# A gated-MLP mixture's u product by one level of Strassen, in 7 of 8 batches

## The chip, the cores and the metric

The kernel runs on one core of one Trainium2 chip. The metric is the device time of one execution in microseconds, the median of the runs shown. "Profile" and "trace" are the record of one such execution.

## What is computed

Attention without a softmax over 8 batches, 8 heads, 576 rows of 64, with an RMS norm; a first mixture (a low-rank token mix, and a channel MLP 512 to 2048 to 512 with ReLU); then the second mixture, which this text is about:

```python
def _moe2_ref(x, w_in, g_ln, w_sg, b_sg, w_out):      # x: 8 x 576 x 512
    h = x @ w_in                                      # 512 x 1024
    h = gelu_tanh(h)
    u, v = (h[..., :512], h[..., 512:])
    v_n = (v - mean(v)) / np.sqrt(var(v) + 1e-06) * g_ln
    v_s = np.einsum('ts,bsd->btd', w_sg, v_n) + b_sg[None, :, None]
    gated = u * v_s
    return (x + gated @ w_out)
```

## The kernel before

Every product in float32 precision is made of three matmuls (`product`, L1611): each operand is split into a high and a low part (ScalarE copies the high one with rounding, VectorE or GpSimd subtracts it for the low one), and hi x hi, hi x lo and lo x hi are summed in PSUM. In the listing of the trace these are L1613, L1614 and L1615.

The first mixture's two big products (to about 836 us) already use one level of Strassen. The second mixture runs batch after batch (b = 2p + par, par the parity). TensorE's order in `iteration` (L1921) is: v product of batch b (`v_product`, tiles of 128 rows, 12 matmuls of 512 columns each; 5 tiles where par is 0, 4 where it is 1, since the 64 rows left over of two batches share a tile), output product of batch b - 1 (`out_product`, 4 tiles while b is odd, 5 while it is even, two banks by turns, so tile i + 2 waits until VectorE has evacuated tile i), u product of batch b (`u_product`: 4 column blocks of 128, 2 halves of 288 rows, 4 chunks), spatial product (`spatial`: 4 column blocks, 28 matmuls of 288 columns each).

The other engines run fixed queues beside it, and a queue is strict: an instruction that waits holds up what is behind it.

- ScalarE: `v_part` (gelu of each v tile into v_act, a ring of three; then the high part vn_hi of the tile before), then in `iteration` (L1075) `x2_high` of the next batch's x, the gelu of u's four column blocks out of PSUM into u_act, and the high parts ga_hi of the gated product.
- VectorE: `v_part` (L1500: statistics of tile j, `normalise` of tile j - 1, `low` of tile j - 2; at its end, behind the last normalise, the evacuation of the output product's tile 0), `evacuate_others`, `x2_transposed` (L1558: transposes xt_in blocks into o_st for the residual), `gate` (L1536: per column block the scale and bias out of PSUM into vs, the mult by u_act, and the low part ga_lo of the block before).
- GpSimd: `inverse_std` per v tile, `x2_low` of the next batch (L765).
- SyncE issues the transfers; `next_batch` (L697) has, in this order: first three xt_in blocks of this batch, the load of the next batch's x (`load_x2`), the output stores of the batch before (each waits for its evacuation), the two tail transfers, the other xt_in blocks (each waits until a buffer has been transposed).

x2_hi and x2_lo stand in two buffers, one per parity; x2_raw, the float32 x, in one. In batch 0 the same steps stand outside the loops, together with the transposes of w_sg.

Of the kernel before, what the change touches and what calls it, by code (L numbers as in the profile page):

```python
# [4 lines left out]
F32 = mybir.dt.float32  # L5
# [5 lines left out]
P = 128  # L11
# [108 lines left out]
def build(nc, q, k, v, g_norm, U, V, w_ch1, w_ch2, w_in, g_ln, w_sg, b_sg, w_out, out):  # L120
# [102 lines left out]
    x2_hi, x2_lo = [None, None], [None, None]  # L223
    o_st = [None] * NO
    cursor[0] = low + 24576
    x2_raw = at("x2_raw", [P, DC, NJ * P], F32)
# [6 lines left out]
    vs = at("vs", [P, 2, S], F32)  # L233
    assert cursor[0] <= hi_off[2]
    cursor[0] = low + 57344
    u_act = at("u_act", [P, DC, S], F32)
    o_st[0] = at("o_st0", [P, D], F32)
    assert cursor[0] <= hb_off[2]
    cursor[0] = hb_off[2]
    x2_lo[0] = at("x2_lo0", [P, DC, NJ * P], F32R)  # L240
    o_st[1] = at("o_st1", [P, D], F32)
    x2_hi[0] = at("x2_hi0", [P, DC, NJ * P], F32R)
# [11 lines left out]
    bias_bc = at("bias_bc", [P, S], F32)  # L254
    assert cursor[0] <= hb_off[1]
# [3 lines left out]
    x2_hi[1] = at("x2_hi1", [P, DC, S], F32R)  # L259
    x2_lo[1] = at("x2_lo1", [P, DC, S], F32R)  # L260
# [3 lines left out]
    with ExitStack() as ctx:  # L264
# [44 lines left out]
        s_x2l, s_x2hi, s_x2lo, s_x2lof = [sem(f"x2_loaded{i}") for i in range(2)], sem("x2_hi_ready"), sem("x2_lo_ready"), sem("x2_lo_first")  # L309
# [62 lines left out]
        def ws_tile(j, n=S):  # L372

            o = (2, 0)[j % 2] * 512
            return psf[:, o:o + n]

# [21 lines left out]
        def _(sp):  # L398
# [174 lines left out]
            def load_x2(p, par):  # L573

                t = (2 * p + par) * S
                if not isinstance(p, int) or p > 0:
                    sp.wait_ge(s_x2lo, 2 * p + par - 1)
                elif par:
                    sp.wait_ge(s_x2lof, 1)
                sp.dma_start(x2_raw[:, :, 0:S], x2T_dram[:, :, bass.ds(t, S)]).then_inc(s_x2l[par], 16)  # L580
                if par == 0:
                    sp.dma_start(x2_raw[:, :, S:], x2T_dram[:, :, bass.ds(t + S + SM, ST)]).then_inc(s_x2l[0], 16)
# [91 lines left out]
            load_x2(0, 0)  # L674
# [16 lines left out]
            load_x2(0, 1)  # L691
# [27 lines left out]
        def _(pool):  # L719
# [45 lines left out]
            def x2_low(p, par):  # L765
                n = (NJ * P, S)[par]
                pool.wait_ge(s_x2hi, 2 * p + par + 1)
                nc.gpsimd.tensor_tensor(x2_lo[par][:, :, 0:n], x2_raw[:, :, 0:n], x2_hi[par][:, :, 0:n].bitcast(F32),
                                        ALU.subtract).then_inc(s_x2lo, 1)
# [21 lines left out]
        def _(act):  # L791
# [91 lines left out]
            def x2_high(p, par, first=False):  # L883
                n = (NJ * P, S)[par]
                act.wait_ge(s_x2l[par], (32, 16)[par] * (p + 1))
                if not first:
                    act.wait_ge(s_umm, DC * (2 * p + par - 1))
                nc.scalar.activation(x2_hi[par][:, :, 0:n], x2_raw[:, :, 0:n], ACT.Copy).then_inc(s_x2hi, 1)


# [156 lines left out]
            def down_tile(t, first=False, last=False):  # L1047
                for n in range(NQ if first else 0, NSL):
                    if first and n in W2_AT:
                        w2_high(W2_AT[n])  # L1050
                    if n == 2 * NQ:
                        first_copied(t)
                    if n < 2:
                        h_relu(t, n + 2)
                    elif n >= NSL - 2 and not last:
                        h_relu(t + 1, n - NSL + 2)
                    if last and n == NSL - 2:
                        x2_high(0, 0, first=True)
# [13 lines left out]
            def us_tile(n):  # L1072
                return ps[:, 4 + 2 * (n % 2):6 + 2 * (n % 2), 0:SH]

            def iteration(p, par, first=False, last=False):  # L1075
                b = 2 * p + par
                if not first and not last:
                    x2_high(*after(p, par))
                for c in range(DC):
                    act.wait_ge(s_umm, DC * b + c + 1)  # L1080
                    if not first:
                        act.wait_ge(s_ga, DC * (b - 1) + c + 1)
                    nc.scalar.activation(u_act[:, c, :].rearrange("p (a m) -> p a m", a=2), us_tile(c),
                                         ACT.Gelu_apprx_tanh).then_inc(s_uact, 1)
                    for j in (WS_AFTER[c] if first else ()):
                        act.wait_ge(s_wsT, j + 1)
                        nc.scalar.activation(ws_hi[:, j, :], ws_tile(j), ACT.Copy).then_inc(s_wshi, 1)
                if first:
                    x2_high(*after(p, par), first=True)
# [44 lines left out]
        def _(dve):  # L1134
# [330 lines left out]
            def x2_low(p, par):  # L1465
                dve.wait_ge(s_x2hi, 2 * p + par + 1)
                for c in range(DC):
                    ins = nc.vector.tensor_tensor(x2_lo[par][:, c, :], x2_raw[:, c, :], x2_hi[par][:, c, :].bitcast(F32), ALU.subtract)
                ins.then_inc(s_x2lof, 1)
# [26 lines left out]
            x2_low(0, 0)  # L1496
# [36 lines left out]
            def us_tile(n):  # L1533
                return ps[:, 4 + 2 * (n % 2):6 + 2 * (n % 2), 0:SH]
# [37 lines left out]
            def evacuate_others(p, par, start=1):  # L1572
                for i in range(start, batch_tiles(par)):
                    evacuate(p, par, i)

# [12 lines left out]
            gate(0, 0, first=True)  # L1588
            with dve.Fori(0, B // 2 - 1) as i:
                v_part(i, 1)  # L1590
                evacuate_others(i, 0)
                x2_transposed(i, 1)
                gate(2 * i + 1, 1)
                v_part(i + 1, 0)
                evacuate_others(i, 1)
                x2_transposed(i + 1, 0)
                dve.wait_ge(s_ost[JM], 32 * (i + 1))
                gate(2 * i + 2, 0)
            v_part(B // 2 - 1, 1)
            evacuate_others(B // 2 - 1, 0)  # L1600
            x2_transposed(B // 2 - 1, 1)
            gate(B - 1, 1)
            for i in range(batch_tiles(1)):
                evacuate(B // 2 - 1, 1, i, bank=i)
# [3 lines left out]
        def _(pe):  # L1608
# [209 lines left out]
            def v_product(p, par, first=False):  # L1818
                if first:
                    pe.wait_ge(s_x2lof, 1)  # L1820
                else:
                    pe.wait_ge(s_x2lo, 2 * p + par)
                for j in range(VB[par], VB[par + 1]):
# [3 lines left out]
                    for c in range(DC):  # L1827
                        ins = product(ps[:, j % 2], [x2_hi[par][:, c, js], x2_lo[par][:, c, js]],
# [16 lines left out]
            def last_out_product(p, par):  # L1845
                tiles = batch_tiles(par)
                for c in range(DC):
                    pe.wait_ge(s_galo, DC * (2 * p + par) + c + 1)
                    for i in range(tiles):
# [5 lines left out]
                        ins = product(ps[:, i], [ga_hi[:, c, js], ga_lo[:, c, js]], [wo_hi[:, c, :], wo_lo[:, c, :]],  # L1855
# [16 lines left out]
            def u_product(b, par, first=False):  # L1872
                for c in range(DC):
                    if c < 2:
                        if not first:
                            pe.wait_ge(s_vs, DC * b + c - 1)
                    else:
                        pe.wait_ge(s_uact, DC * b + c - 1)
                    for h in range(2):
                        dst = ps[:, 4 + 2 * (c % 2) + h, 0:SH]  # L1880
                        hs = slice(h * SH, (h + 1) * SH)
                        for d in range(DC):
                            ins = product(dst, [wu_hi[:, d, c * P:(c + 1) * P], wu_lo[:, d, c * P:(c + 1) * P]],
                                          [x2_hi[par][:, d, hs], x2_lo[par][:, d, hs]], d == 0, d == DC - 1)
                        if h == 1:
                            ins.then_inc(s_umm, 1)
                        if first and (c, h) in WS_AT:
                            w_sg_transposed(WS_AT[c, h])

            def spatial(p, par):  # L1890
                b = 2 * p + par
                pe.wait_ge(s_vnlo, NCP * p + VB[par + 1])
                for c in range(DC):
                    if c < 2:
# [4 lines left out]
                    for h in range(2):  # L1899
                        dst = ps[:, 4 + 2 * (c % 2) + h, 0:SH]  # L1900
# [15 lines left out]
            u_product(0, 0, first=True)  # L1916
# [4 lines left out]
            def iteration(p, par):  # L1921
                v_product(p, par)
                out_product(*before(p, par))
                u_product(2 * p + par, par)
# [32 lines left out]
```

## Time and profile before

| | us |
|---|---|
| median of 3 runs | 1268.24 (1268.18 to 1269.29) |
| profiled execution | 1268.39 |
| its span | 1266.4 |
| TensorE busy | 1244.6 (98%) |
| VectorE busy | 862.8 (68%) |
| ScalarE busy | 541.4 (43%) |
| GpSimd busy | 107.6 (8%) |

PE is TensorE's matmuls, PEld its weight loads, which overlap them; DVE is VectorE, ACT ScalarE, POOL GpSimd, SP SyncE. A matmul's shown duration overlaps the next one's, so the pace of TensorE is read from the starts. Times in the trace count from the start of the span. A number in brackets behind a row is how long the engine stood idle before it, with what ended that.

### The profile page before, as it was taken

How to read it: one execution, taken by the hardware profiler on the slowest of the kernel's cores; microseconds unless marked ns; L12 is line 12 of the kernel's file. 1: busy time of each engine (PE TensorE's matmuls, PEld its weight loads, DVE VectorE, ACT ScalarE, POOL GpSimd, SP SyncE). 2: the span in 40 equal slices, each digit the busy share in tenths (PEclk: the TensorE clock that was granted, in tenths of full speed). 3: DMA queues.
4: the chain of work that ended last, by engine and by line, in shares of the span. 5: the costliest groups of instructions: out<-in, count | busy, mean ns of one | idle time of the engine just before them, and what ended most of it. 6: DMA issues, size and time to landing. Idle time of an engine off the chain costs nothing.

```text
span 1266.4 us, 21681 instructions
## 1 busy us (share of the span) xinstructions
PE 1244.6 (98%) x8213; PEld 1204.7 (95%) x8213; DVE 862.8 (68%) x1292; ACT 541.4 (43%) x882; POOL 107.6 (8%) x116
## 2 busy tenths in 40 slices
PE   6999999999999999999999999999999999999998
PEld 6899999999999999999999999999899898998997
DVE  5987667676767668988898888976543544445444
ACT  4674555554545446454454444543222312223120
POOL 5430000000000000000000000012202202022000
PEclk9999999999999999999999999999999999999999
DMA  9687878878787587464362728362324142250221
GB/s 209 184 219 206 202 210 216 219 195 204 217 218 207 155 278 269 152 212 171 129 215 83 261 70 286 106 178 55 88 63 94 56 95 58 66 120 33 50 59 42
DMA packets 364119, 194.81 MB, mean 154 GB/s; under 512 B 259568, under 2 KB 334592, under 8 KB 364048
## 3 DMA queue, kind: packets, MB, share of 16 engines
q1 hardware_dynamic: 359760, 188.72, 53.3%
q0 software_dynamic: 1728, 4.57, 1.5%
q8 instruction: 44, 0.72, 0.2%
q10 hardware_dynamic: 2560, 0.59, 0.2%
q14 instruction: 27, 0.22, 0.1%
HBM read 117.14 MB, written 74.58 MB: 151 GB/s over the span
## 4 chain that ended last, share of the span: by engine, by line
PE 93%; DVE 4%; DMA 1%; issue 1%; POOL 1%; ACT 0%; ACTq 0%; DVEq 0%
PE ps L1613 28%; PE ps L1615 28%; PE ps L1614 28%; PE ps L1634 2%; PE ps L1645 2%; PE ps L1653 1%; PE ps L1905 1%; PE ps L1908 1%; DVE w L1188 1%; PE ps L1618 1%; PE ps L1671 1%; DMA w_raw<-in_moe_w_ch 1%; PE ps L1647 0%; DVE h_st L1228 0%; POOL w_raw L746 0%
## 5 line engine op out<-in xcount | busy, mean ns | idle before, releaser
L1613 PE MATMUL ps<-x_hi,w 128*128 128x288 f32 x896 | 268.0, 299 | 3.4 <-DVE h_st L1228 2.3
L1614 PE MATMUL ps<-x_lo,w 128*128 128x288 f32 x896 | 264.3, 295 | 0.0
L1615 PE MATMUL ps<-x_hi,w 128*128 128x288 f32 x896 | 263.9, 295 | 0.0
L1613 PE MATMUL ps<-r_hi,w_hi 128*128 128x384 f32 x672 | 224.6, 334 | 0.2 <-DVE r_lo L1399 0.2
L1615 PE MATMUL ps<-r_hi,w_lo 128*128 128x384 f32 x672 | 224.5, 334 | 0.0
L1614 PE MATMUL ps<-r_lo,w_hi 128*128 128x384 f32 x672 | 224.5, 334 | 0.0
L1006 ACT ACTIVATE r_hi<-hb 128x768 fp32r<-128x768 f32 x168 | 142.3, 848 | 166.5 <-PE ps L1615 161.1
L1613 PEld LDWEIGHTS ps<-x_hi,w 128*128 128x128 f32 x896 | 168.1, 188 | 5.9 <-DVE h_st L1228 3.0
L1615 PEld LDWEIGHTS ps<-x_hi,w 128*128 128x128 f32 x896 | 168.6, 188 | 0.0
L1614 PEld LDWEIGHTS ps<-x_lo,w 128*128 128x128 f32 x896 | 168.4, 188 | 0.0
L1401 DVE TENSOR_TENSOR r_lo<-hb,r_hi 128x768 fp32r<-128x768 f32 x120 | 114.7, 958 | 30.5 <-ACT r_hi L1006 30.5
L1613 PEld LDWEIGHTS ps<-r_hi,w_hi 128*128 128x128 f32 x672 | 126.1, 188 | 0.6 <-DVE r_lo L1399 0.6
L1615 PEld LDWEIGHTS ps<-r_hi,w_lo 128*128 128x128 f32 x672 | 126.1, 188 | 0.0
L1614 PEld LDWEIGHTS ps<-r_lo,w_hi 128*128 128x128 f32 x672 | 126.1, 188 | 0.0
L881 ACT ACTIVATE h_st<-ps 128x576 f32<-128x576 f32 x128 | 81.1, 647 | 61.4 <-PE ps L1615 59.4
L1228 DVE TENSOR_TENSOR h_st<-ps,h_st 128x576 f32<-128x576 f32 x96 | 72.1, 754 | 37.3 <-PE ps L1615 36.8
L1550 DVE SCALAR_TENSOR_TENSOR vs<-ps,glcol,bias_bc 128x576 f32<-128x576 f32 x32 | 26.1, 817 | 88.4 <-PE ps L1908 88.4
L1613 PE MATMUL ps<-ws_hi,vn_hi 128*128 128x288 f32 x256 | 75.8, 296 | 0.7 <-DVE ws_hi L1584 0.7
L1613 PE MATMUL ps<-x_hi,wu_hi 128*128 128x288 f32 x256 | 75.8, 296 | 0.0
L1615 PE MATMUL ps<-x_hi,wu_lo 128*128 128x288 f32 x256 | 75.5, 295 | 0.0
L1614 PE MATMUL ps<-ws_lo,vn_hi 128*128 128x288 f32 x256 | 75.4, 295 | 0.0
L1615 PE MATMUL ps<-ws_hi,vn_lo 128*128 128x288 f32 x256 | 75.4, 294 | 0.0
(170 smaller groups left out, 2342.3 us busy)
## 6 DMA issues: line engine op xcount, KB each, us to landing
hT_scratch<-h_st SPq DMA_DIRECT2D x64, 576.0 KB, 4.2
hb<-hT_scratch SPq DMA_DIRECT2D x24, 1536.0 KB, 7.3
uT_scratch<-x_raw SPq DMA_DIRECT2D x32, 288.0 KB, 4.7
x_st<-uT_scratch SPq DMA_DIRECT2D x24, 384.0 KB, 3.6
x2T_scratch<-x_st SPq DMA_DIRECT2D x24, 384.0 KB, 5.7
x_raw<-x2T_scratch SPq DMA_DIRECT2D x8, 1152.0 KB, 5.8
xt_in<-x2T_scratch SPq DMA_DIRECT2D x144, 64.0 KB, 2.5
y_scratch<-y SPq DMA_DIRECT2D x26, 320.0 KB, 3.1
```

The source lines that it names most:

```text
L881: nc.scalar.activation(h_st[:, g % 2, :, {0: 0, 1: 3, 2: 1, 6: 2}[idx], :], ps[:, o:o + 2, 0:SH], ACT.Copy).then_inc(s_cp, 1)
L1006: nc.scalar.activation(r_hi[:, n % RING], piece(h_source(i), q_), ACT.Relu if i in (3, 6) else ACT.Copy).then_inc(s_hhi, 1)
L1188: nc.vector.tensor_tensor(w1[a // 2][:, a % 2, 1, i], w1_raw[min(a // 2, 1)][:, a if a < 2 else a - 2, 1, i], w1[a // 2][:, a % 2, 0, i].b ...
L1228: nc.vector.tensor_tensor(c, ps[:, o:o + 2, 0:SH], c, ALU.add).then_inc(s_ad, 1)
L1401: ins = nc.vector.tensor_tensor(lo, x, hi, ALU.subtract)
L1550: nc.vector.scalar_tensor_tensor(vs[:, c % 2, :].rearrange("p (a m) -> p a m", a=2), us_tile(c), glcol[:, c:c + 1], bias_bc[:].rearrange(" ...
L1613: mm(dst, ws[0], xs[0], start=first, stop=False, skip_group_check=chained)
L1614: mm(dst, ws[0], xs[1], start=False, stop=False, skip_group_check=chained)
L1615: return mm(dst, ws[1], xs[0], start=False, stop=last, skip_group_check=chained)
L1618: return mm(dst, src, identF[:], is_transpose=True, start=start, stop=stop)
L1634: ins = mm(ps[:, bx, at_:at_ + P], k_raw[n][:, j], v_raw[n][:, :, j, :], start=(j == 0), stop=(j == NJ - 1))
L1645: ins = mm(ps[:, bx, j * P:(j + 1) * P], qT[:, j], kv[:], start=True, stop=True)
```

## The change

Batch 0 keeps its u product (with the two pairs of banks swapped). In batches 1 to 7 the product of x (512 x 576, transposed) and the u half of w_in (512 x 512) is cut in 2 x 2 blocks of 256 x 288 and 256 x 256 and made of 7 block products, in the variant with shared sums. Four sums of weight blocks are made once, four sums of x blocks per batch, in place in x2_raw, by VectorE; each is split into high and low. The 7 products use three pairs of banks (X = 4 and 5, Y = 0 and 1, Z = 6 and 7) in the order X Y X Z X Y X: ScalarE copies three of them to u_act, TensorE goes on adding in the same bank, VectorE adds three more from PSUM to u_act, and the gelu is then taken in place in u_act, the last from PSUM.

x2_hi and x2_lo now stand in one buffer, whose room pays for the sums. So x2 of the next batch is loaded in two halves after products 4 and 6 of this one, and its high and low parts are made during the spatial product.

The core of the diff (declarations, waits renamed only, and the new placing of buffers left out):

```diff
@@ SyncE @@
+                elif not (isinstance(b, int) and b == 0):
+                    sp.wait_ge(s_sp, NI * (b - 2) + (5, 7)[half])
+                cs = slice(2 * half, 2 * half + 2)
+                sp.dma_start(x2_raw[:, cs, 0:S], x2T_dram[:, cs, bass.ds(t, S)]).then_inc(s_x2l[par][half], 16)
...
             def next_batch(p, par, q_, qpar, last=False):
                 load_first_blocks(p, par)
-                if not last:
-                    load_x2(*after(p, par))
                 store_out(q_, qpar)
                 stack_tail(p, par)
                 load_other_blocks(p, par)
+                if not last:
+                    load_x2(*after(p, par), 0)
+                    load_x2(*after(p, par), 1)
@@ ScalarE: batches 1 to 7, behind v_part @@
+                    for n in range(4):
+                        t_high(b, n)
+                    act.wait_ge(s_ga, DC * b)
+                    for idx in range(3):
+                        u_copied(b, idx)
+                    for n in range(4):
+                        u_gelu(b, n)
                 if not first and not last:
                     x2_high(*after(p, par))
...
@@ VectorE @@
+            def evacuate_others(p, par, b):
+                for i in range(1, batch_tiles(par)):
+                    if i < 3:
+                        t_low(b, 2 * i - 2)
+                        t_low(b, 2 * i - 1)
                     evacuate(p, par, i)
+            def t_sums(b):
+                b11, b12, b21, b22 = (x2_raw[:, k:k + 2, h * SH:(h + 1) * SH] for k in (0, 2) for h in range(2))
+                dve.wait_ge(s_x2lo, 2 * b)
+                nc.vector.tensor_tensor(b11, b12, b11, ALU.subtract).then_inc(s_ts, 1)
+                dve.wait_ge(s_ts, 4 * (b - 1) + 1)
+                nc.vector.tensor_tensor(b12, b22, b12, ALU.subtract).then_inc(s_ts, 1)
+                dve.wait_ge(s_ts, 4 * (b - 1) + 2)
+                nc.vector.tensor_tensor(b22, b22, b11, ALU.subtract).then_inc(s_ts, 1)
+                dve.wait_ge(s_ts, 4 * (b - 1) + 3)
+                nc.vector.tensor_tensor(b21, b21, b22, ALU.subtract).then_inc(s_ts, 1)
+            def u_added(b, n):
+                dve.wait_ge(s_sp, NI * (b - 1) + n + 4)
+                dve.wait_ge(s_ucp, 3 * (b - 1) + n + 1)
+                c = u_part(*((0, 0), (1, 1), (0, 1))[n])
+                o = U_BANK[n + 3]
+                nc.vector.tensor_tensor(c, ps[:, o:o + 2, 0:SH], c, ALU.add).then_inc(s_uad, 1)
...
             x2_transposed(0, 0, first=True)
+            wu_sums()
...
             gate(0, 0, first=True)
+            for n in range(4):
+                wu_sum_low(n)
+            t_sums(1)
+            def batch(p, par, q_, qpar):
+                b = 2 * p + par
+                v_part(p, par)
+                evacuate_others(q_, qpar, b)
+                x2_transposed(p, par)
+                for n in range(3):
+                    u_added(b, n)
             with dve.Fori(0, B // 2 - 1) as i:
+                batch(i, 1, i, 0)
                 gate(2 * i + 1, 1)
+                t_sums(2 * i + 2)
+                batch(i + 1, 0, i, 1)
                 dve.wait_ge(s_ost[JM], 32 * (i + 1))
                 gate(2 * i + 2, 0)
+                t_sums(2 * i + 3)
@@ TensorE @@
+            def u_product(p, par):
+                b = 2 * p + par
+                for idx in range(NI):
+                    if idx == 0:
+                        pe.wait_ge(s_slo, 4)
+                        pe.wait_ge(s_vs, DC * b)
+                    elif idx == 1:
+                        pe.wait_ge(s_vact, NCP * p + VB[par + 1])
+                    elif idx == 2:
+                        pe.wait_ge(s_ucp, 3 * (b - 1) + 1)
+                    elif idx == 4:
+                        pe.wait_ge(s_ucp, 3 * (b - 1) + 3)
+                    elif idx == 5:
+                        pe.wait_ge(s_ucp, 3 * (b - 1) + 2)
+                    elif idx == 6:
+                        pe.wait_ge(s_uad, 3 * (b - 1) + 2)
+                    if idx in (1, 2, 4, 6):
+                        pe.wait_ge(s_tlo, 4 * (b - 1) + (1, 2, 4, 6).index(idx) + 1)
+                    for m in range(2):
+                        cs = slice(m * P, (m + 1) * P)
+                        for d in range(2):
+                            ins = product(ps[:, U_BANK[idx] + m, 0:SH], [u_weights(idx, d, cs, 0), u_weights(idx, d, cs, 1)],
+                                          [u_moving(idx, d, 0), u_moving(idx, d, 1)], d == 0 and idx in (0, 1, 3), d == 1, chained=idx != 3)
+                    ins.then_inc(s_sp, 1)
```

The spatial product's first column block now waits for the first of VectorE's additions (it takes bank pair Z), its second for all four gelus. `wu_sums` are four sums of 512 elements, each waiting for the one before, as in `t_sums`; ScalarE and VectorE then split them (`wu_sum_high`, `wu_sum_low`). `x2_low` on GpSimd works in two halves, and `t_high`, `t_low` split each sum of x, 576 elements wide.

## Rows read from the trace of the kernel before

**Rows 1.** The page: TensorE's busy time; the chain that ended last, by engine.

```profile
PE 1244.6 (98%) x8213; PEld 1204.7 (95%) x8213; DVE 862.8 (68%) x1292; ACT 541.4 (43%) x882; POOL 107.6 (8%) x116
...
PE 93%; DVE 4%; DMA 1%; issue 1%; POOL 1%; ACT 0%; ACTq 0%; DVEq 0%
```

**Rows 2.** Busy time by stretch, batch 5: engines, PE clock, DMA share, GB/s.

```profile
1094.99:1105.89 10.90, 10.90 (x50) 9.02 (x49) 6.90 (x15) 3.01 (x5) 1.60 (x3) 1.00 0.00 0
1105.89:1116.78 10.89, 10.89 (x50) 9.01 (x49) 6.35 (x13) 4.74 (x5) 5.04 (x3) 1.00 0.19 72
1116.78:1129.50 12.72, 12.72 (x98) 12.72 (x97) 3.92 (x6) 1.95 (x3) 1.97 (x1) 1.00 0.51 99
1129.50:1144.34 14.84, 14.84 (x114) 14.84 (x113) 6.21 (x10) 2.99 (x7) 0.00 (x0) 1.00 0.49 118
```

**Rows 3.** Timeline of VectorE, batches 5 and 6: start, duration, instruction.

```profile
1096.72 1.59 DVE L1540 TENSOR_TENSOR ga_lo<-vs,ga_hi 128x576 fp32r<-128x576 f32 x2
1098.64 0.69 DVE L1504 BATCH_NORM_STATS2 bn<-v_act 128x6 f32<-128x512 f32 x1 [0.33 <-ACT v_act L1108]
...
1102.50 0.54 DVE L1513 TENSOR_SCALAR v_act<-v_act,mv,rs 128x512 f32<-128x512 f32 x1
1104.32 0.69 DVE L1504 BATCH_NORM_STATS2 bn<-v_act 128x6 f32<-128x512 f32 x1 [1.29 <-ACT v_act L1108]
...
1109.96 0.69 DVE L1570 TENSOR_TENSOR o_st<-ps,o_st 128x512 f32<-128x512 f32 x1
...
1111.76 0.69 DVE L1570 TENSOR_TENSOR o_st<-ps,o_st 128x512 f32<-128x512 f32 x1
...
1146.08 1.75 DVE L1540 TENSOR_TENSOR ga_lo<-vs,ga_hi 128x512 fp32r<-128x512 f32 x4
...
1162.29 0.68 DVE L1570 TENSOR_TENSOR o_st<-ps,o_st 128x512 f32<-128x512 f32 x1
```

**Rows 4.** Timeline of ScalarE, batch 5: the loop's v_act, the last vn_hi.

```profile
1103.71 0.58 ACT L1108 ACTIVATE v_act<-ps 128x512 f32<-128x512 f32 x1
...
1110.08 0.63 ACT L1117 ACTIVATE vn_hi<-v_act 128x512 fp32r<-128x512 f32 x1 [0.43 <-DVE v_act L1513]
```

**Rows 5.** Timeline of VectorE: last evacuation, transposes that waited, batches 5 and 6.

```profile
1116.97 0.69 DVE L1570 TENSOR_TENSOR o_st<-ps,o_st 128x512 f32<-128x512 f32 x1 [2.03 <-PE ps L1615]
...
1123.64 0.71 DVE L1564 STREAM_TRANSPOSE o_st<-xt_in 128x512 f32<-128x512 f32 x1 [4.17 <-DMA xt_in<-x2T_scratch]
1125.96 0.71 DVE L1564 STREAM_TRANSPOSE o_st<-xt_in 128x512 f32<-128x512 f32 x1 [1.60 <-DMA xt_in<-x2T_scratch]
...
1171.77 0.69 DVE L1570 TENSOR_TENSOR o_st<-ps,o_st 128x512 f32<-128x512 f32 x1 [2.03 <-PE ps L1615]
...
1179.32 0.71 DVE L1564 STREAM_TRANSPOSE o_st<-xt_in 128x512 f32<-128x512 f32 x1 [5.05 <-DMA xt_in<-x2T_scratch]
```

**Rows 6.** Tile x_raw, first mixture: a 576-wide sum of x, min/median/max ns.

```profile
L1195 DVE TENSOR_TENSOR x_raw<-x_raw x8: 753/757/759, 36.8 to 416.9; 128x576 f32<-128x576 f32 x8
```

**Rows 7.** Timelines of VectorE, GpSimd, TensorE, batch 0.

```profile
877.04 0.78 DVE L1550 SCALAR_TENSOR_TENSOR vs<-ps,glcol,bias_bc 128x576 f32<-128x576 f32 x1
877.85 1.73 DVE L1553 TENSOR_TENSOR vs<-vs,u_act 128x576 f32<-128x576 f32 x1
...
873.79 5.18 POOL L768 TENSOR_TENSOR x_lo<-x_raw,x_hi 128x2304 fp32r<-128x2304 f32 x1 [15.38 <-ACT x_hi L888]
...
879.27 0.29 PE L1613 MATMUL ps<-ws_hi,vn_hi 128*128 128x288 f32 x1
```

**Rows 8.** The page's groups: copy and addition out of PSUM in the first mixture.

```profile
L881 ACT ACTIVATE h_st<-ps 128x576 f32<-128x576 f32 x128 | 81.1, 647 | 61.4 <-PE ps L1615 59.4
L1228 DVE TENSOR_TENSOR h_st<-ps,h_st 128x576 f32<-128x576 f32 x96 | 72.1, 754 | 37.3 <-PE ps L1615 36.8
```

**Rows 9.** The page's DMA issues; timeline of GpSimd: load and low part of x2.

```profile
x_raw<-x2T_scratch SPq DMA_DIRECT2D x8, 1152.0 KB, 5.8
...
1113.03 5.72 POOL L768 TENSOR_TENSOR x_lo<-x_raw,x_hi 128x2560 fp32r<-128x2560 f32 x1 [3.64 <-ACT x_hi L888]
```

More of the change, by code:

```diff
@@ L881, in copied, with x2_high_first, x2_high, u_copied @@
                 nc.scalar.activation(h_st[:, g % 2, :, {0: 0, 1: 3, 2: 1, 6: 2}[idx], :], ps[:, o:o + 2, 0:SH], ACT.Copy).then_inc(s_cp, 1)
-            def x2_high(p, par, first=False):
-                n = (NJ * P, S)[par]
[L885 to L888, printed above, removed]
+            def x2_high_first():
+                for half in range(2):
+                    act.wait_ge(s_x2l[0][half], 32)
+                nc.scalar.activation(x2_hi[:], x2_raw[:], ACT.Copy).then_inc(s_x2hi, 1)
+            def x2_high(p, par):
+                n = (NJ * P, S)[par]
+                for half in range(2):
+                    cs = slice(2 * half, 2 * half + 2)
+                    act.wait_ge(s_x2l[par][half], (32, 16)[par] * (p + 1))
+                    nc.scalar.activation(x2_hi[:, cs, 0:n], x2_raw[:, cs, 0:n], ACT.Copy).then_inc(s_x2hi, 1)
+            def u_copied(b, idx):
+                act.wait_ge(s_sp, NI * (b - 1) + idx + 1)
+                nc.scalar.activation(u_part(*((0, 0), (1, 1), (0, 1))[idx]), ps[:, U_BANK[idx]:U_BANK[idx] + 2, 0:SH], ACT.Copy).then_inc(s_ucp, 1)
+            def u_gelu(b, n):
+                dst = u_part(*((0, 0), (1, 1), (0, 1), (1, 0))[n])
+                if n < 3:
+                    act.wait_ge(s_uad, 3 * (b - 1) + n + 1)
+                    nc.scalar.activation(dst, dst, ACT.Gelu_apprx_tanh).then_inc(s_uact, 1)
+                else:
+                    act.wait_ge(s_sp, NI * b)
+                    nc.scalar.activation(dst, ps[:, UX:UX + 2, 0:SH], ACT.Gelu_apprx_tanh).then_inc(s_uact, 1)
+            def t_high(b, n):
+                act.wait_ge(s_ts, 4 * (b - 1) + T_SUM[n])
+                nc.scalar.activation(t_hi[:, n], t_slot(x2_raw, n), ACT.Copy).then_inc(s_thi, 1)
+            def wu_sum_high(n):
+                act.wait_ge(s_sw, 4)
+                dst = s_hi[:, n] if n < 3 else wu_hi[:, 0:2, DH:D]
+                nc.scalar.activation(dst, s_slot(n), ACT.Copy).then_inc(s_shi, 1)
             def load_q(m):
@@ L1057, in down_tile @@
                     if last and n == NSL - 2:
-                        x2_high(0, 0, first=True)
+                        x2_high_first()
                     h_high(t, n)
@@ L1072, in us_tile, with first_u @@
             def us_tile(n):
-                return ps[:, 4 + 2 * (n % 2):6 + 2 * (n % 2), 0:SH]
+                return ps[:, 6 - 2 * (n % 2):8 - 2 * (n % 2), 0:SH]
+            def first_u():
+                for c in range(DC):
+                    act.wait_ge(s_umm, c + 1)
+                    nc.scalar.activation(u_act[:, c, :].rearrange("p (a m) -> p a m", a=2), us_tile(c),
+                                         ACT.Gelu_apprx_tanh).then_inc(s_uact, 1)
+                    for j in WS_AFTER[c]:
+                        act.wait_ge(s_wsT, j + 1)
+                        nc.scalar.activation(ws_hi[:, j, :], ws_tile(j), ACT.Copy).then_inc(s_wshi, 1)
+                x2_high(0, 1)
+                for n in range(4):
+                    wu_sum_high(n)
             def iteration(p, par, first=False, last=False):
                 b = 2 * p + par
+                if first:
+                    first_u()
+                else:
+                    if isinstance(b, int) or par:
+                        act.wait_ge(s_slo, 4)
+                    for n in range(4):
[5 more added lines that the diff above has]
+                        u_gelu(b, n)
                 if not first and not last:
                     x2_high(*after(p, par))
[L1079 to L1089, printed above, removed]
                 for c in range(DC):
@@ L1495, in _ @@
             down_tile(NTILE - 1, last=True)
-            x2_low(0, 0)
+            x2_low_first()
             x2_added(NTILE - 1, NI - 1)
@@ L1893, in spatial @@
                 for c in range(DC):
-                    if c < 2:
+                    if c == 0 and not (isinstance(b, int) and b == 0):
+                        pe.wait_ge(s_uad, 3 * (b - 1) + 1)
+                    elif c < 2:
                         pe.wait_ge(s_uact, DC * b + c + 3)
@@ L1915, in _ @@
             pe.wait_ge(s_x2, NA2 * NTILE)
[L1916 removed]
+            u_product_first()
             pe.wait_ge(s_wsb, 1)
```

141 lines of the change are left out of this document (93 added, 48 removed).

## The prediction

> **What bounds it.** The page first: TensorE is busy 98% of the span and the chain that ended last is 93% TensorE; of the second mixture no other engine stands in the chain with more than 1% [rows 1]. Then the busy time of one batch of that mixture, stretch by stretch (batch 5; the others repeat it): v product 10.90 us, output product 10.89, u product 12.72, spatial product 14.84, each filled by TensorE to the last hundredth, at a granted clock of 1.00 (2.4 GHz) [rows 2]. So time leaves only where matmuls leave, and any new wait of TensorE is added whole. What I need next is how much room the queues of the other engines have around it: the timelines of VectorE and ScalarE [rows 3, 4], and of the transposes that stand ahead of the new additions [rows 5].
>
> **What is removed.** A u product has 96 matmuls, 4 columns x 2 halves x 4 chunks x 3 terms, in 12.72 us [rows 2]: 0.1325 us each, which also fits the spatial product (112 in 14.84). Seven block products of 12 make 84. 12 x 0.1325 = 1.59 us a batch, 7 batches: **-11.1 us**. One block product takes 1.59 us.
>
> **What is added, VectorE.** Per batch four sums of x, four low parts, three additions out of PSUM. A 576-wide sum of x in SBUF takes 0.757 us in the first mixture [rows 6]; each waits for the one before, so 0.79 apiece (the gate's mult starts 0.03 after its vs ends, as 877.85 stands to 877.04 + 0.78 [rows 7]), 3.16 for four. Where nothing waits, an instruction starts 0.09 before the one ahead ends (the three from 1109.96 to 1111.76, 0.69 each [rows 3]); so a low part of 0.75 issues every 0.66, an addition from PSUM of 0.754 [rows 8] every 0.67. That is some 8 us more on an engine busy about half of these 49 us [rows 2]. In total it fits. It doesn't where it is placed.
>
> *(1) The sums stand between the gate and the v part.* Count from the start of a v product. In batch 5 the gate before it ends at 3.3 (1096.72 + 1.59 - 1094.99), the statistics of tile 0 start at 3.65, normalise(0) at 7.51 [rows 3]. With the sums VectorE reaches tile 0 at 3.2 + 3.16 = 6.4; two rounds of statistics take 2 x 1.13, normalise(0) starts at 8.7: 1.2 late. It is not won back: normalise(0) releases vn_hi, that v_act of tile 2 (1103.71), that statistics of tile 2 (1104.32), a loop which already goes round in 3.0 us against 2.73 of TensorE's tile [rows 3, 4]. So the evacuation of output tile 0, which VectorE does behind the last normalise, is 1.2 late. It ended at 15.66; TensorE wants it after two output tiles, at 10.90 + 5.45 = 16.35 [rows 2, 3]. Room 0.69, and 0.1 for the signal (an estimate between 0.03, v_act's end to statistics, and 0.19, a tile's end to its evacuation [rows 3 to 5]): TensorE stands 0.6 us. In even batches the gate ends 0.2 later (1146.08 + 1.75) and the room is 13.63 + 5.45 - (1162.97 - 1144.34) = 0.45: 1.0 us.
>
> *(2) Two low parts stand ahead of the evacuation of tile 1.* Evacuation 1 starts 1.80 after evacuation 0 [rows 3]; 1.32 more makes 3.12, its end 3.81. TensorE began tile 2 at 0.79 and wants it at 3.52; with the signal 0.4 us. ScalarE is no help or harm: vn_hi at 1110.08 is followed by the high parts, 0.6 each, in place of x2_high (which moves away), ready when asked for [rows 4]. The next two low parts precede evacuation 2, which has a whole tile of room. So (1) and (2) are 1.0 us in odd batches, 1.5 in even ones.
>
> *(3) The additions stand behind the transposes.* Product 6 overwrites the bank that addition 1 reads, and VectorE comes to the additions only after x2_transposed. From the end E of the output product (1116.78 in batch 5, 1171.58 in batch 6: 0.19 before the start of its last evacuation), the blocks of tile 3 are transposed at E + 6.86 and of tile 4 at E + 9.18 in odd batches, of tile 3 at E + 7.74 in even ones, each after a wait for a transfer [rows 5]. SyncE sends for them only after the last output store and the tails, which all count from E, so nothing moves them. VectorE is free at E + 9.8 or 8.4; two additions 0.67 + 0.75, signal 0.1: E + 11.3 or 9.9. Product 6 could start at 6 x 1.59 = E + 9.54. Stall **1.8 us** odd, **0.3** even. Before, the u product had no reader on VectorE, and this lateness was covered.
>
> *Without (1) to (3) the stage would be as the first mixture's*, where copies of 0.647 us and additions of 0.754 [rows 8] are inside a product's 1.59; so ScalarE's three copies and the gelus cost nothing. The spatial product starts in the bank that addition 0 frees, and its second column comes 3.7 us after product 6, behind the last gelu.
>
> *(4) x2 in one buffer.* The loads of the next x2 go behind load_other_blocks in SyncE's queue and wait for products 4 and 6; queued behind them are the 12 loads of the next first blocks, wanted only after the next output product, some 30 us on. Second half after the end U of the u product: landing at most 5.8 (the whole one's time), ScalarE 1.2, GpSimd 2.9 (half of 5.72) [rows 9]: U + 10, asked for at U + 14.84. Nothing, with 4.8 us of room. ScalarE's x2_high stands ahead of ga_hi, so up to U + 7; the gate needs its low part by U + 9. Nothing.
>
> **What is added once.** Between the transposes and the gate of batch 0 come the weight sums, 4 x 0.72 (512 wide). VectorE is there at 877.04, but GpSimd is in x2_low; the mult at 877.85 took 1.73 us instead of 0.76 and ended 0.6 after GpSimd's (873.79 + 5.18) [rows 7]. In halves x2_low starts a microsecond sooner and ends near 878.1: sums done 880.9, first gate step out of PSUM 881.65. TensorE wants that bank at 879.16 (its third column started at 879.27 [rows 7]): **2.6 us**. Without the clash it would be 1.7. The Trainium skill, SBUF — State Buffer, Who interferes with whom, says a VectorE instruction with two SBUF inputs fully blocks on a GpSimd instruction that reads SBUF. The 1.73 us agrees; by that rule the first weight sum would end 0.1 later than I take it, and in the steady batches the additions out of PSUM wouldn't be touched. Then behind gate 0 the low parts of the weights, about 2.6 us, go in front of the sums of x: by (1) batch 1 comes to tile 0 at 3.2 + 2.6 + 3.16 = 9.0 and to normalise(0) at 11.2, 3.7 late; TensorE stands 3.7 - 0.69 + 0.1 = 3.1, with (2) 3.5.
>
> **The sum.** Stalls: batch 0 2.6; batch 1 3.5 + 1.8; batches 3, 5, 7 3 x (1.0 + 1.8) = 8.4; batches 2, 4, 6 3 x (1.5 + 0.3) = 5.4. Together 21.7; less 11.1: **+10.6 us**. The profiled execution took 1268.39 (span 1266.4), 0.15 over the median of 1268.24, which is nothing here: 1279.0. What lies behind the last spatial product is unchanged.
>
> **Rivals.**
> *The cover holds, all 11.1 us come in* (other side): VectorE would have to win back 1.2 us in the v part, and blocks land 2 us sooner. For it: it idles 1.3 us before the statistics. Against: that idling is inside a loop. 1268.24 - 11.1 = 1257.1. Chance 0.07. It turns faster than before once the stalls together are under 11.1.
> *Only the sums of x are absorbed*, while additions still come behind the transposes and batch 0 pays: 2.6 + 4 x 1.8 + 3 x 0.3 = 10.7 against 11.1: 1267.8, no change. For it: rooms of 0.69 and 0.45 are near the delay. Against: the loop at 3.0 us, as above. Chance 0.07.
> *x2 comes late as well*: if both halves, the blocks and the stores queue up, more than 4.8 us late in (4), the v product waits in each of 6 batches, 1 to 2 us: 1285 to 1291. Against: transfer engines half free then [rows 2]. Chance 0.10.
> *A sum of x costs other than 0.79*: 0.70 gives 2.5 us less, 0.90 3 us more; within the forecast, which has 0.76.
>
> **How the numbers follow.** The likeliest is 1279.0. Its own range by the sums' price (-2.5, +3), blocks a microsecond sooner (-4 in the four odd batches), no clash (-0.9): 1272 to 1284. With part of the late x2 case the range is 1271 to 1286. 0.2% is 2.5 us, about what a measurement here can tell. Faster 0.08, same 0.08, slower 0.84.
>
> **What would show it.** Waits of TensorE, 0.7 us in all in this stage before, should name: VectorE's evacuation some 14 times (0.4 to 3.3 us), its addition from PSUM in product 6 (1.8 and 0.3 in turn), its gate in batch 0 (2.6). A u product should be 12.9 and 11.4 us by turns, an output product 11.9 and 15.1 (13.6 without stalls). The first number that would break it: statistics of tile 2 not late by 1.2 us, or tile 4's transpose well before E + 9.

## The result, and the profile after

The changed kernel takes 1286.53 us, median of 4 runs (1283.94 to 1291.27), against 1268.76 (1268.18 to 1270.13): ratio 1.0143, 95% interval 1.0112 to 1.0174. The forecast was 1279.0 in a range of 1271 to 1286: the sign was right and nearly every place, the size too small by 7.5 us, and the time lies half a microsecond outside the range. The profiled execution took 1286.33, 17.9 more than that of the kernel before.

TensorE's waits in the second mixture, in total, times, longest (L1720 is the addition out of PSUM, L1666 the evacuation of an output tile, L1646 the gate's first step, L1769 the first matmul of a product):

```profile
PE ps L1769 <- DVE u_act L1720: 10.8, 7, 3.0
PE ps L1769 <- DVE o_st L1666: 5.5, 6, 2.9
PE ps L1769 <- DVE vs L1646: 2.2, 1, 2.2
PE ps L1769 <- DVE ws_hi L1730: 0.7, 1, 0.7
```

Only the last line was there before. The three above it are the three places that the prediction names. (In batches 1 to 6 the view shows one wait per output product; the second, at evacuation 1, and both of batch 7 are under its limit and are read from the length of the stretch.)

Busy time by stretch, columns as in [rows 2]. First the spatial product of batch 0, then u and spatial product of batch 1, output and u product of batch 3, u and spatial product of batch 7 (the row of this u product begins 0.11 us behind its first matmul; the product takes 14.88):

```profile
872.39:889.85 17.46, 15.22 (x113) 14.99 (x113) 11.91 (x16) 6.21 (x9) 5.32 (x2) 1.00 0.39 61
915.24:930.30 15.06, 12.06 (x86) 11.83 (x85) 5.89 (x9) 3.97 (x6) 0.00 (x0) 0.95 0.55 129
930.30:945.97 15.67, 15.67 (x114) 15.67 (x113) 6.25 (x10) 5.42 (x9) 5.90 (x2) 0.94 0.50 93
1012.38:1024.24 11.86, 11.51 (x50) 8.85 (x48) 9.79 (x20) 4.79 (x8) 1.56 (x2) 1.00 0.11 44
1024.24:1037.33 13.09, 11.36 (x85) 11.13 (x84) 5.89 (x9) 3.97 (x6) 0.00 (x0) 1.00 0.62 150
1236.05:1250.82 14.77, 11.82 (x85) 11.59 (x84) 5.89 (x9) 3.97 (x6) 0.00 (x0) 0.96 0.39 84
1250.82:1266.65 15.83, 15.83 (x114) 15.83 (x113) 6.20 (x10) 2.99 (x7) 0.00 (x0) 0.93 0.01 1
```

Against the 12.72 us of [rows 2] the u product of batch 3 is longer although it has 84 matmuls and not 96: its matmuls fill 11.13, the rest is a stand. And the column after GpSimd's shows what the prediction had not thought of: in batches 1 and 7 the granted clock is not 1.00, and a spatial product, in which TensorE never waits, takes 15.67 and 15.83 us where those of batches 2 to 6 take 14.85.

All stretches, each from the first matmul of a product to the first of the next; a stand is the length less that of the matmuls (output 10.88 or 13.60, u 11.13):

| batch | output product, stand | u product, beyond its matmuls | spatial, beyond 14.85 |
|---|---|---|---|
| 1 | 3.6 | 3.9 | 0.8 |
| 2 | 1.4 | 0.9 | 0 |
| 3 | 1.0 | 2.0 | 0 |
| 4 | 1.4 | 0.8 | 0 |
| 5 | 1.0 | 1.95 | 0 |
| 6 | 1.4 | 0.4 | 0 |
| 7 | 0.85 | 3.75 | 1.0 |
| forecast | 3.5; 1.0 odd, 1.5 even | 1.8 odd, 0.3 even | 0 |

The u column of batches 1 and 7 contains 1.2 us of the lower clock. With 2.5 us in the spatial product of batch 0 (forecast 2.6) all comes to 28.6 us; less 11.1 for the matmuls is 17.5, and the second mixture began 0.65 later than in the profile of before: within 0.3 of the 17.9 between the profiled executions. These 0.65 us are no effect of the change that could be shown: in the eight profiles of this document the second mixture begins anywhere from 840.3 to 843.2 us.

### The profile page after: what moved, and what is told of

Its sections match the earlier page's. It is cut to its first block and busy times, and to the rows that moved or that the text cites. A ratio compares the mean times of both kernels' runs of the same rounds, so it can differ in the third digit from the quotient of the medians.

```text
span 1284.7 us, 21859 instructions
## 1 busy us (share of the span) xinstructions
PE 1244.1 (97%) x8129; PEld 1197.3 (93%) x8129; DVE 921.4 (72%) x1380; ACT 574.5 (45%) x942; POOL 108.9 (8%) x123
## 5 line engine op out<-in xcount | busy, mean ns | idle before, releaser
L1769 PE MATMUL ps<-x_hi,w 128*128 128x288 f32 x896 | 267.9, 299 | 3.2 <-DVE h_st L1324 2.1
L1769 PE MATMUL ps<-r_hi,w_hi 128*128 128x384 f32 x672 | 224.6, 334 | 0.3 <-DVE r_lo L1495 0.3
L1769 PEld LDWEIGHTS ps<-x_hi,w 128*128 128x128 f32 x896 | 168.1, 188 | 5.7 <-DVE h_st L1324 2.9
L1769 PEld LDWEIGHTS ps<-r_hi,w_hi 128*128 128x128 f32 x672 | 126.1, 188 | 0.6 <-DVE r_lo L1495 0.6
L1769 PE MATMUL ps<-ws_hi,vn_hi 128*128 128x288 f32 x256 | 76.7, 299 | 3.0 <-DVE vs L1646 2.2
L1646 DVE SCALAR_TENSOR_TENSOR vs<-ps,glcol,bias_bc 128x576 f32<-128x576 f32 x32 | 26.2, 818 | 72.7 <-PE ps L2087 72.7
L1769 PE MATMUL ps<-wo_hi,ga_hi 128*128 128x512 f32 x144 | 57.7, 401 | 6.4 <-DVE o_st L1666 5.5
```

Source lines behind the costliest of these rows:

```text
L1646: nc.vector.scalar_tensor_tensor(vs[:, c % 2, :].rearrange("p (a m) -> p a m", a=2), us_tile(c), glcol[:, c:c + 1], bias_bc[:].rearrange(" ...
L1769: mm(dst, ws[0], xs[0], start=first, stop=False, skip_group_check=chained)
```

## The experiments

Theory A: the loss is nothing but TensorE standing behind the order of VectorE's queue at three places, (1) and (2) in the output product, (3) at product 6, and the weights' sums in batch 0, plus, since the trace of after, the clock that falls behind a long stand. Rival B: VectorE has not the time, and a stand moved away comes back elsewhere. Rival C: the single x2 buffer and its transfers cost it. The first five experiments are the changed kernel with one thing moved or added, the last makes the three moves in VectorE's queue together.

### The additions ahead of the last transposes

```diff
-                x2_transposed(p, par)
+                x2_transposed(p, par, tiles=range(NXT))
                 for n in range(3):
                     u_added(b, n)
+                x2_transposed(p, par, tiles=range(NXT, batch_tiles(par)))
```

> One thing is moved in VectorE's queue of the changed kernel: its three additions out of PSUM now stand between the transposes of tiles 0 to 2 and those of tiles 3 and 4, which wait for transfers. Theory A (the loss is TensorE standing behind VectorE's order): product 6 no longer waits, each u product of batches 1 to 7 takes 11.1 to 11.3 us instead of 15.07, 12.01, 13.09, 11.92, 13.08, 11.52, 14.88; with no stand of 3 us there the clock stays at 1.00, so the spatial products of batches 1 and 7 fall from 15.67 and 15.83 to 14.85. Together 15.5 us less: about 1271. The stands in the output products stay as they are. Rival B (VectorE has not the time, wherever its work stands): the transposes now come late, the gate is late, and TensorE waits in the spatial product for what it no longer waits for in product 6; time 1281 or more. Rival C (the loss lies in the x2 transfers of the single buffer): no change of more than 2 us.

1274.28 us (1270.82 to 1274.93), ratio to before 1.0043 (1.0027 to 1.006). The forecast of about 1271 is met by the profiled execution alone, which took 1270.82; the three others took 1274 to 1275, at a mean granted clock of 0.994 to 0.995 where the profiled one has 0.997. Waits of TensorE:

```profile
PE ps L1770 <- DVE o_st L1666: 5.5, 6, 2.9
PE ps L1770 <- DVE vs L1646: 2.2, 1, 2.2
```

The wait for the addition has gone, all seven. Timeline of VectorE in batch 3 (L1720 addition, L1660 transposes, L1646 gate):

```profile
1019.44 1.89 DVE L1660 STREAM_TRANSPOSE o_st<-xt_in 128x512 f32<-128x512 f32 x3
1025.27 0.76 DVE L1720 TENSOR_TENSOR u_act<-ps,u_act 128x576 f32<-128x576 f32 x1 [3.93 <-PE ps L1772]
1026.84 0.76 DVE L1720 TENSOR_TENSOR u_act<-ps,u_act 128x576 f32<-128x576 f32 x1 [0.82 <-PE ps L1772]
1028.44 0.76 DVE L1720 TENSOR_TENSOR u_act<-ps,u_act 128x576 f32<-128x576 f32 x1 [0.84 <-PE ps L1772]
1029.12 1.30 DVE L1660 STREAM_TRANSPOSE o_st<-xt_in 128x512 f32<-128x512 f32 x2
1033.82 0.82 DVE L1646 SCALAR_TENSOR_TENSOR vs<-ps,glcol,bias_bc 128x576 f32<-128x576 f32 x1 [3.41 <-PE ps L2088]
```

Now VectorE waits for TensorE and not the other way; the late transposes still leave 3.4 us before the gate. Every u product takes 11.11 to 11.12 us, every spatial product from batch 1 on 14.85. Rival B falls at this place, and so does C: the x2 loads, their high and low parts are where they were in the queues, and neither a u nor a spatial product of batches 1 to 7 stands. In this profile the clock fell once all the same, behind the stand in batch 0 (spatial product 18.85 us instead of 17.46).

### The sums of x spread over the v part

```diff
                 end = VB[par + 1]
+                if not first:
+                    t_sum(2 * p + par, 0)
                 for j in range(VB[par], end):
                     stats(j)
                     if j > VB[par]:
                         normalise(j - 1)
                     if j > VB[par] + 1:
                         low(j - 2)
+                    if not first and j < VB[par] + 3:
+                        t_sum(2 * p + par, j - VB[par] + 1)
```

(and `t_sums` behind the gates left out)

> One thing is moved in the changed kernel: the four sums of x of a batch no longer stand together ahead of the v part; one stands there, the other three behind the statistics and low parts of v tiles 0, 1 and 2, where VectorE waited 1.5, 1.3 and 0.7 us before the change. Theory A: the delay of the v part goes, evacuation 0 is on time, and with it the stand at evacuation 1: output products of 10.9 and 13.6 us instead of 11.9 and 15.0 in batches 2 to 7; in batch 1 the weights' low parts (2.6 us) still stand ahead, so 12.9 instead of 14.5. 8.5 us less: about 1278. The u products keep their waits. Rival B (VectorE has not the time): the gaps are too short, the delay comes back at the last v tile, output products stay at 11.5 and 14.5 or more: 1284 or more.

1277.12 us (1276.21 to 1278.3), ratio 1.0062 (1.0045 to 1.0078). Waits of TensorE:

```profile
PE ps L1767 <- DVE u_act L1721: 9.1, 7, 2.7
PE ps L1767 <- DVE vs L1650: 2.2, 1, 2.2
PE ps L1767 <- DVE o_st L1670: 1.2, 1, 1.2
```

Output products: 10.88, 10.91 and 10.88 us in batches 3, 5 and 7, 13.76 to 13.81 in the even ones, 12.80 in batch 1. So step (1) is right, and step (2) too in this sense: two low parts ahead of evacuation 1 cost nothing once evacuation 0 is on time (0.2 us is left in even batches, where the room was 0.45). The three sums fit the gaps. Two things were not as expected. The u products' waits did not stay, they fell from 10.8 to 9.1 us in all, since tile 4 was transposed 0.3 to 0.5 us sooner in the odd batches. And the clock fell three times in this profile and not twice: behind the stand in batch 0 (2.24 us; spatial product 18.99), and at product 6 of batches 1 and 7, though the stands there were down to 2.7 and 2.5.

### The weights' sums early

```diff
                 nc.vector.tensor_tensor(ws_lo[:, j, :], ws_tile(j), ws_hi[:, j, :].bitcast(F32),
                                         ALU.subtract).then_inc(s_wslo, 1)
+                if 1 <= j <= 4:
+                    wu_sum(j - 1)
...
-            x2_transposed(0, 0, first=True)
-            wu_sums()
+            x2_transposed(0, 0, first=True, tiles=range(NXT))
+            for n in range(4):
+                wu_sum_low(n)
+            x2_transposed(0, 0, first=True, tiles=range(NXT, JM))
```

(ScalarE makes the weights' high parts ahead of x2's, and `wu_sum_low` behind gate 0 is gone)

> One thing is moved in the changed kernel: the four weight sums are made in VectorE's gaps between the low parts of w_sg, their high parts ahead of x2's, their low parts while VectorE waits for the last block of x2 of batch 0, not ahead of and behind the gate of batch 0. Theory A: the stand of 2.24 us in the spatial product of batch 0 goes (17.46 us become 14.96), and batch 1 reaches its v part 2.6 us sooner, its output product falls from 14.48 to 11.9: 5.1 us less, about 1281, and one fall of the clock may go with it if the stand in product 6 of batch 1 ends shorter. Rival (the clash with GpSimd's x2_low, which now runs later, during the gate): the spatial product of batch 0 keeps 1 to 2 us of its stand; 1283.

1281.27 us (1279.02 to 1282.92), ratio 1.0101 (1.0084 to 1.0118). The time is as forecast, but only half of it for the reasons forecast. The output product of batch 1 came down to 11.89 us, as expected. The stand in batch 0 did not go, it is 3.0 us instead of 2.2, and the clock fell behind it (spatial product 19.70). Timelines of VectorE and GpSimd, then of VectorE in the changed kernel:

```profile
873.30 4.54 DVE L1706 TENSOR_TENSOR s_lo<-s_raw,s_hi 128x256 fp32r<-128x256 f32 x6
877.77 3.12 DVE L1708 TENSOR_TENSOR wu_lo<-s_raw,wu_hi 128x512 fp32r<-128x512 f32 x1
880.81 0.70 DVE L1660 STREAM_TRANSPOSE o_st<-xt_in 128x512 f32<-128x512 f32 x1
...
874.80 5.54 POOL L821 TENSOR_TENSOR x_lo<-x_raw,x_hi 128x1152 fp32r<-128x1152 f32 x2 [16.50 <-ACT x_hi L946]
...
893.09 2.10 DVE L1709 TENSOR_TENSOR s_lo<-s_raw,s_hi 128x256 fp32r<-128x256 f32 x6
895.10 0.69 DVE L1711 TENSOR_TENSOR wu_lo<-s_raw,wu_hi 128x512 fp32r<-128x512 f32 x1
```

In the changed kernel, where GpSimd had nothing to do at that time, the six took 2.10 us and the one 0.69. Beside GpSimd's x2_low they take 4.54 and 3.12: the clash that the prediction priced at a microsecond can cost 4.9. It is the rival named in the expectation, and it cost more than the rival said. What made up for it is the u and spatial products of batches 1 and 7, together 5.2 us shorter: their stands at product 6 were 1.96 and 1.89 us here instead of 3.0 and 2.95, and after neither did the clock fall. In this profile tile 4 was transposed about 1.0 us sooner in both batches than in the changed kernel. The edit touches nothing in batch 7, so there at least it is no effect of it that could be shown: the pace of the transfers differs from profile to profile.

### Filler matmuls in the stand

```diff
                     elif idx == 6:
+                        if par:
+                            pe.wait_ge(s_oev, NCP * p + 3)
+                            for n in range(12):
+                                mm(ps[:, 2, 0:SH], wu_hi[:, 0, 0:P], x2_hi[:, 2, 0:SH], start=True, stop=True)
                         pe.wait_ge(s_uad, 3 * (b - 1) + 2)
```

> Nothing is moved; in batches 1, 3, 5, 7 TensorE runs 12 more matmuls of 288 columns into a free bank between product 5 and the wait ahead of product 6 (their result is not used). They take 1.59 us of a stand of 1.7 to 3.0 us. This asks what the granted clock costs. Theory A1 (the clock falls because TensorE stands 3 us): with the stand cut to half the clock stays at 1.00, the matmuls behind it take 0.13 us from start to start and not 0.24, the spatial products of batches 1 and 7 are 14.85 instead of 15.67 and 15.83; 3 us less, about 1283, and the runs scatter less than 1283.9 to 1291.3. Rival A2 (the fall has another cause, as the u product's shorter rows or the load): the clock falls all the same and the time is unchanged within 1 us.

1282.91 us (1279.54 to 1287.29), ratio 1.0115 (1.0085 to 1.0145). At the two places the clock stayed as A1 says: the wait at product 6 of batch 1 was 0.69 us, the spatial products of batches 1 and 7 took 14.84 and 14.86 us. That the filler did it is not shown. Its u products of batches 1 and 7, 13.65 and 13.10 us, are 2.5 and 2.0 longer than 84 matmuls, where the changed kernel's stands, without the part of the clock, made 3.3 and 3.2: the transfers were sooner here too. In the experiment before this one, 2.2 and 2.1 us without any filler were not followed by a fall either. The case that the clock follows stands rests on the count at the end of this document. What the run does show is that A2's cause, the u product's shorter rows, is not needed: in the same profile the clock fell at two other stands that the filler doesn't touch, in the spatial product of batch 0 (2.23 us) and in the output product of batch 1 (2.87), where it had stayed up in the profile of after. The median is 3.6 us lower; the scatter, which A1 wanted to shrink, did not.

### The blocks of the last tiles ahead of the tails

```diff
-                stack_tail(p, par)
                 load_other_blocks(p, par)
+                stack_tail(p, par)
```

> The changed kernel with one thing moved in SyncE's queue: the transfers of the xt_in blocks of tiles 3 and 4 go ahead of the two tail transfers, which take 0.5 and 0.6 us to issue. Theory A (what sets the stand at product 6 is SyncE's queue from the last output store on, and VectorE's transposes behind it): the blocks land 1.1 us sooner, the u products of batches 3 and 5 fall from 13.1 to 12.0, of 1 and 7 by 1.1 to some 13.8, of the even ones by what they stand, 0.4 to 0.9, to 11.2; stands under 2.2 us let the clock be at some places. 5 to 9 us less: about 1279. Rival (the landing is set by the transfers themselves, not by when they are issued): under 2 us less, 1285.

1276.6 us (1275.57 to 1278.11), ratio 1.0058 (1.0041 to 1.0076). The u products are 13.18, 11.12, 11.82, 11.11, 12.06, 11.12 and 12.98 us: in even batches nothing is left of the stand, in odd ones 1.0 to 1.3 us less in batches 3 and 5. So SyncE's queue sets when product 6 may start. Two transfers of together 1.1 us to issue, moved, and the median is 10 us lower (5 to 9 were expected): in the profile 7 of shorter stands and 3.0 of a clock that no longer fell at product 6, less 1.1 for a fall in the output product of batch 1 (15.61 us). That is some 9 us; another 1.5 lie ahead of the stage, where the two kernels are the same.

### All moved

The additions and the sums of x as above; the weight sums between the low parts of w_sg, but their low parts in two gaps of gate 0 and behind it, out of the way of GpSimd:

```diff
                     if c > 0:
                         low(c - 1)
+                    if first and c in (1, 2):
+                        wu_sum_low(c - 1)
...
-            for n in range(4):
+            for n in range(2, 4):
                 wu_sum_low(n)
```

> All three moves in one kernel: additions ahead of the last transposes, sums of x spread over the v part, and the weight sums in the gaps between the low parts of w_sg. The weights' low parts are not ahead of the gate this time (there they clashed with GpSimd's x2_low and took 4.5 and 3.1 us instead of 2.1 and 0.7): two stand in gaps of the gate of batch 0, two behind it. Theory A (all that was lost was TensorE standing behind VectorE's order, and the work itself fits): no stand is left over 0.2 us, u products 11.11, output products 10.9 and 13.8, spatial product of batch 0 14.96, no fall of the clock in this stage. Before minus 11.1 plus some 0.7: 1258.3, faster than the kernel before by 0.8%. Rival B (the block products or the single x2 buffer cost something of their own, which the stands hid): some product is longer than its matmuls by 0.5 us or more, and the time is 1262 or more.

**1259.34 us** (1257.2 to 1261.47, 6 runs) against 1268.52 (1267.56 to 1272.26, 11 runs) of the kernel before: ratio 0.9917, interval 0.9902 to 0.9932. The only wait of TensorE that this view has left in the stage, and the busy times of two whole batches, 4 and 5, from v product to v product:

```profile
PE ps L1768 <- DVE ws_hi L1732: 0.7, 1, 0.7
```

```profile
1038.20:1091.56 53.36, 53.36 (x318) 48.41 (x317) 32.88 (x59) 18.08 (x28) 9.55 (x7) 1.00 0.30 71
1091.56:1139.34 47.78, 47.78 (x294) 43.98 (x293) 31.52 (x54) 17.36 (x28) 9.30 (x6) 1.00 0.35 82
```

TensorE is busy in all of an even batch (53.36 us; before, 54.80 from the start of batch 6 to that of batch 7) and an odd one (47.78; before, 49.35, the sum of [rows 2]). VectorE is busy 66% of the odd batch, which was 47% before, and TensorE has no wait for it here that the view shows. The block products cost their matmuls and no more: every u product takes 11.11 to 11.12 us. Rival B falls: the work fits, it was only queued ahead of work that TensorE wanted sooner. What is left against 11.1 us gained: 0.55 in the output product of batch 1 and 0.2 in each even batch. These 0.55 are a hair over the mark that rival B set for a single product, but it is not a block product, and the time is 2.7 us under B's. The profile bears the sum out: from the start of the second mixture to the last spatial product's end it is 10.1 us shorter than that of before. The fall of the clock has gone from the stage with the stands.

## Why the prediction was right and where it was wrong

- **What bounds it, and the 11.1 us.** Right. A u product takes 11.11 us instead of 12.72, seven times, once nothing stands in the way.
- **(1) the sums ahead of the v part.** Right in mechanism and size. Normalise(0) was to be 1.2 us late (it was 1.1) and the loop at 3.0 us was not to win it back. Timeline of VectorE in batch 3 of after (the batch's v product starts at 1001.47, so these are 8.6 and 16.7; [rows 3] has 7.5 and 15.7 with evacuation 0 ending):

```profile
1007.76 0.69 DVE L1600 BATCH_NORM_STATS2 bn<-v_act 128x6 f32<-128x512 f32 x1
...
1010.05 0.54 DVE L1609 TENSOR_SCALAR v_act<-v_act,mv,rs 128x512 f32<-128x512 f32 x1
1011.87 0.69 DVE L1600 BATCH_NORM_STATS2 bn<-v_act 128x6 f32<-128x512 f32 x1 [1.28 <-ACT v_act L1204]
...
1017.50 0.69 DVE L1666 TENSOR_TENSOR o_st<-ps,o_st 128x512 f32<-128x512 f32 x1
...
1020.64 0.69 DVE L1666 TENSOR_TENSOR o_st<-ps,o_st 128x512 f32<-128x512 f32 x1
```

- **(2) low parts ahead of evacuation 1.** Right: evacuation 1 starts 3.14 us after evacuation 0 (3.12 forecast), and (1) and (2) together stood 1.0 and 1.4 us a batch (1.0 and 1.5).
- **(3) the additions behind the transposes.** The mechanism is right, and the experiments on the order of the additions and on SyncE's queue both show it. The size was wrong, and this is the step that failed first: 12.5 us in seven batches (the u column above, less 1.2 of clock) where 8.1 were forecast; 3 of the 4.4 us are in batches 1 and 7. I took the delay from batches 5 and 6 alone, wrote that nothing moves it, and priced a spread only downwards (-4). But it is a chain of eight transfers that SyncE issues one by one, and their pace varies: counted from E, the end of the output product, tile 4 is transposed at 9.3 in batches 3 and 5, at 10.6 and 10.5 in batches 1 and 7. Reading every batch of before would not have shown it: tile 4 stands there at 8.9 to 9.4 in all four odd batches. Timeline of SyncE in batch 7 of before, then in batches 5 and 7 of after:

```profile
1223.37 4.34 SPq L595 DMA_DIRECT2D xt_in<-x2T_scratch  x8
...
1133.13 4.23 SPq L642 DMA_DIRECT2D xt_in<-x2T_scratch  x8
...
1238.40 5.70 SPq L642 DMA_DIRECT2D xt_in<-x2T_scratch  x8
```

  The same eight take 1.4 to 1.5 us longer in batch 7 of after; in batches 1 and 7 there is a pause of 1.1 and 1.3 us between two of them, with a transfer of the instruction queues near it. These batches stand outside SyncE's loop. That the pause is the fetch of new code was not tried: its cause stays open. It is no fixed delay of these batches either: in the experiments with the sums spread, the weights early and the filler, tile 4 comes at 9.6 to 10.3 in batch 1 and at 9.3 to 10.1 in batch 7. In even batches tile 3 came at 8.2, 8.1 and 7.7; I had used 7.74, the soonest of the three even batches of before (7.75 to 7.96).
- **(4) the single x2 buffer.** Right: nothing. In the changed kernel and in all six experiments every v product starts at once.
- **The weights, batch 0 and batch 1.** Right: 2.5 for 2.6, 3.6 for 3.5. The first sum, beside x2_low, took 1.56 us.
- **The clock.** Missing: the second step that failed is a term put at nothing without a reason. The sum took every stand at its own length. Matmuls behind the stand in batch 7, from the timeline of TensorE:

```profile
1248.57 0.40 PE L1769 MATMUL ps<-t_hi,wu_hi 128*128 128x288 f32 x1 [2.95 <-DVE u_act L1720]
...
1249.06 0.29 PE L1769 MATMUL ps<-t_hi,wu_hi 128*128 128x288 f32 x1
1249.19 0.29 PE L1770 MATMUL ps<-t_lo,wu_hi 128*128 128x288 f32 x1
...
1250.10 0.44 PE L1769 MATMUL ps<-t_hi,wu_hi 128*128 128x288 f32 x1
1250.34 0.44 PE L1770 MATMUL ps<-t_lo,wu_hi 128*128 128x288 f32 x1
```

  From start to start they take 0.13 us, then 0.24 us (1.2 GHz and not 2.4) until 1252.9, then 0.13 again. About 14 matmuls at 0.11 more each: 1.5 us for a fall, twice in this profile, 3.0 us.

The miss of 7.5 us is thus, within 0.2, 4.4 from (3), 3.0 from the clock, 0.65 of a later start of the stage, less 0.4 in batch 0 and the output products. Without the 3.0 of the clock the time would have been inside the range, (3) or not. The range itself was drawn too loosely: above 1279.0 its terms give 3 us, 1282, and it says 1284 and then 1286 for a case that did not happen; that the result came so near its edge is luck. The rival of 1285 to 1291, x2 late as well, had the time and not the reason.

## What to carry to other kernels

Where TensorE is never idle, any new operand of another engine is free only if it stands in that engine's queue behind what TensorE wants first: look for the waits that the engine has already, and put the new work into them, not ahead of them. Keep what waits for a transfer behind what TensorE waits for. And when stands are added up, price a long one above its length, since the clock may fall behind it (here behind 10 of 14 stands of 2.2 to 3.0 us, at 1.1 to 1.5 us each). A delay that comes from a chain of transfers gets a spread to both sides: here 8.9 to 9.4 us from E before the change became 9.3 to 10.6 behind it.

## What was not expected of the hardware

- The clock behind a stand. In six profiles of kernels with these stands (the changed one and five experiments), TensorE stood 2.2 to 3.0 us 14 times in the second mixture, and the granted clock fell behind 10 of them; behind none of the stands under 2 us. The same stand of 2.2 us in batch 0 was followed by a fall in three profiles and not in two. One fall cost 1.4 to 1.5 us in 288-wide matmuls (spatial product of batch 0 18.85 to 18.99 us with it, 17.46 and 17.45 without), 1.1 in the 512-wide output product (15.52 and 15.61 against 14.48). In the two profiles without such stands, before and all moved, it did not fall between the start of the second mixture and its last spatial product's end. This count ties the falls to the stands; what decides between fall and no fall at the same length stays open. It would explain why the changed kernel's runs scatter over 7 us: the longest, 1291.27, has a mean clock of 0.993, the others 0.994 and 0.996. But in the runs that were not profiled no stretch can be looked at.
- Six subtractions of 256 elements with both inputs in SBUF took 4.54 us beside a GpSimd subtraction and 2.10 without one, a single one of 512 elements 3.12 against 0.69. The instruction of VectorE that reads PSUM and, beside a column of one element per row, one operand in SBUF was not lengthened: the gate's first step took 0.78 while x2_low ran [rows 7]. This agrees with the rule of the Trainium skill cited above (SBUF — State Buffer, Who interferes with whom); its price depends on how long GpSimd's instruction still runs (the 3.12 us began at 877.77, GpSimd's ended at 880.34, and VectorE's 0.55 behind it).
